# First pair by banks A, B, D, C; short units' operands at the end of their slots; one wait and one turn moved into the first unit's second half

## The reference

```
qn = q / (norm(q, over rows) + 1e-6);  kn = k / (norm(k, over rows) + 1e-6)
a  = softmax(kn^T @ qn / tau)                  # 256 x 256, for each of B = 2 batches
x  = v @ a                                     # 12032 rows of 256
x  = (sigmoid(x @ w_gate) * (x @ w_val)) @ w_out    # d_ff = 1536
h  = x @ w2_in                                 # d_ff = 2048
out = (h - tanh(h)) @ w2_out
```

## Time and profile before

| | before |
|---|---|
| three runs | 2207.38, 2208.68, 2209.26 us, median 2208.68 |
| the profiled execution's own time | 2208.35 us |
| its span, first to last instruction | 2206.4 us |
| granted TensorE clock, mean | 0.999 |
| PE busy | 2189.4 us (99%) |
| VectorE, ScalarE, GpSimd busy | 1549.3, 1276.1, 1153.4 us |
| DMA traffic | 439.46 MB |

### The profile page before, as it was taken

The page is one execution under the profiler, slowest core; times in us unless marked ns, Lnnn a source line. Parts: engine busy times, 40 slices in busy tenths (PEclk is TensorE's granted clock), DMA queues, the critical chain, the costliest instruction groups (busy, mean ns, idle before and its releaser), DMA issues.

```text
span 2206.4 us, 33618 instructions
## 1 busy us (share of the span) xinstructions
PE 2189.4 (99%) x11664; PEld 1908.3 (86%) x11664; DVE 1549.3 (70%) x2933; ACT 1276.1 (58%) x2336; POOL 1153.4 (52%) x970
## 2 busy tenths in 40 slices
PE   8999999999999999999999999999999999999998
PEld 6887988888888898899998898888888889889998
DVE  6879866866775776686586586586586677577566
ACT  5644664665565565565565465465466456556555
POOL 3475653564465464365374365356356446446434
PEclk9999999999999999999999999999999999999999
DMA  9988476476367357457557547546536536635644
GB/s 335 323 284 316 168 218 224 141 237 210 127 211 241 125 182 227 169 178 237 199 187 228 185 168 222 175 140 216 191 134 212 185 134 202 207 124 182 232 143 151
DMA packets 286473, 439.46 MB, mean 199 GB/s; under 512 B 208096, under 2 KB 214496, under 8 KB 286304
## 3 DMA queue, kind: packets, MB, share of 16 engines
q1 hardware_dynamic: 279184, 409.82, 56.5%
q0 software_dynamic: 5264, 27.27, 3.2%
q10 hardware_dynamic: 1856, 0.23, 0.1%
HBM read 386.14 MB, written 51.12 MB: 198 GB/s over the span
## 4 chain that ended last, share of the span: by engine, by line
PE 95%; DMA 2%; POOL 1%; DVE 1%; issue 1%; ACT 0%; SPq 0%; ACTq 0%; DVEq 0%; POOLq 0%
PE up L1610 53%; PE x_acc L1610 21%; PE acc L1610 19%; PE x_acc L1636 3%; DMA qk_in<-in_k 1%; DMA w_sums<-g 0%; POOL g L694 0%; POOL g L689 0%; DVE g_lo L1323 0%; POOL vt_lo L705 0%; POOL vt_hi L705 0%; POOL x_lo L705 0%; POOL g L687 0%; SPq L438 0%; ACT g L877 0%
## 5 line engine op out<-in xcount | busy, mean ns | idle before, releaser
L739 POOL TENSOR_TENSOR g<-t_sums,g 128x512 fp32r<-128x512 f32 (+1 forms) x384 | 502.5, 1325 | 371.1 <-ACT g L1026 371.0
L729 POOL TENSOR_TENSOR g_lo<-func_out,g_hi 128x512 fp32r<-128x512 f32 (+1 forms) x253 | 313.8, 1269 | 570.6 <-ACT g_hi L961 570.4
L1610 PE MATMUL up<-vt_hi,ring 128*128 128x512 f32 (+1 forms) x1848 | 562.6, 386 | 0.0
L1610 PEld LDWEIGHTS up<-vt_hi,ring 128*128 128x128 f32 x1848 | 347.3, 188 | 62.8
L1610 PE MATMUL up<-vt_lo,ring 128*128 128x512 f32 (+1 forms) x924 | 358.5, 388 | 0.3
L1336 DVE TENSOR_TENSOR held<-up,held 128x512 f32<-128x512 f32 (+1 forms) x132 | 89.7, 679 | 366.8 <-PE up L1610 366.8
L1026 ACT ACTIVATE g<-t_sums 128x512 fp32r<-128x512 f32 (+1 forms) x384 | 237.8, 619 | 157.2 <-DVE t_sums L1419 156.9
L1610 PE MATMUL x_acc<-g,ring 128*128 128x256 f32 (+1 forms) x2304 | 304.4, 282 | 0.0
L1610 PE MATMUL up<-x_lo,in_w_hi 128*128 128x512 f32 (+1 forms) x768 | 298.3, 388 | 1.1 <-DVE x_lo L1379 1.1
L1610 PE MATMUL up<-x_hi,in_w_lo 128*128 128x512 f32 (+1 forms) x768 | 297.7, 388 | 0.0
L1610 PE MATMUL up<-x_hi,in_w_hi 128*128 128x512 f32 (+1 forms) x768 | 296.2, 386 | 0.0
(11 more groups left out here) (258 smaller groups left out, 3617.3 us busy)
## 6 DMA issues: line engine op xcount, KB each, us to landing
ring<-w_sums SPq DMA_DIRECT2D x192, 896.0 KB, 4.6
ring<-u_records SPq DMA_DIRECT2D x132, 896.0 KB, 6.1
d_ring<-d_records SPq DMA_DIRECT2D x70, 512.0 KB, 6.3
qk_in<-in_q SPq DMA_DIRECT2D x29, 384.0 KB, 4.5
qk_in<-in_k SPq DMA_DIRECT2D x29, 384.0 KB, 6.0
u_records<-g POOLq DMA_DIRECT2D x12, 896.0 KB, 10.7
v_in<-in_v SPq DMA_DIRECT2D x160, 64.0 KB, 2.4
out_rows<-out_sb SPq DMA_DIRECT2D x160, 64.0 KB, 2.2
```

What stands on the lines that cost most here:

```text
L729: pool.tensor_tensor(g1_lo[:, i, 0:w], func_out[:, i, 0:w], g1_hi[:, i, 0:w].bitcast(F32), ALU.subtract).then_inc(g_lo_made, 2 if last and ...
L739: pool.tensor_tensor(lo[:, cut, 0:half], t_sums[:, first - T1:first - T1 + 2, 0:half], hi[:, cut, 0:half].bitcast(F32), ALU.subtract).then ...
L1610: mm = pe.matmul(psum, a, b, start=start and n == 0, stop=stop and n == 2, skip_group_check=shared_bank)
```

## The change

The banks of the first pair are taken in the order A, B, D, C, on all engines: VectorE's products, ScalarE's high parts, GpSimd's low parts, and the opening of the next pair's gate on TensorE, which becomes M1, M6, M5, M7, M2 in place of M1, M5, M6, M7, M2. In a short unit the operands that TensorE streams (v, x of both blocks, g) lie in the last 448 (or 224) columns of their slots; the columns that the other engines read from and the PSUM columns stay. The turn of the second half of v for unit 1 goes from step j = 10 of unit 0's first half to pair k = 1 of its second half. The wait for `u_s_stored[5]` goes from before the second half to `hi_of_vt_sums(0, 1)`, at k = 13, which is what overwrites the staged parts.

```diff
+    def tail(w):
+        return slice(W - w, W)
+    def half_tail(half):
+        return slice(W // 2 - half, W // 2)
...
-    FIRST_ORDER = [A_, D_, C_, B_]
+    FIRST_ORDER = [A_, B_, D_, C_]
...
+    SEAM_M6, SEAM_M5 = 2, 3
...
-        NEXT_V_TURNS = [3, 10]
+        FIRST_V_TURN, LATE_V_TURN = 3, 1
...
-                sp.dma_start(v_in[g * Q:(g + 1) * Q, h, 0:w // Q, :],
+                sp.dma_start(v_in[g * Q:(g + 1) * Q, h, TB - w // Q:TB, :],
...
-                    pool.tensor_tensor(g1_lo[:, i, 0:w], func_out[:, i, 0:w],
-                                       g1_hi[:, i, 0:w].bitcast(F32), ALU.subtract
+                    pool.tensor_tensor(g1_lo[:, i, tail(w)], func_out[:, i, 0:w],
+                                       g1_hi[:, i, tail(w)].bitcast(F32), ALU.subtract
... (the same for g1_hi, x2_hi, x2_lo with tail(w), and for the parts of g2 with half_tail(half))
             def hi_of_vt_sums(t, n):
                 act.wait_ge(vt_summed, 4 * (t + 1))
+                if t == 0 and n == 1:
+                    act.wait_ge(u_s_stored[FOLDS - 1], 32)
...
                 hi_of(t, 0, A_, w)
+                hi_of(t, 0, B_, w)
                 hold_a(gate_steps, gate_copied, n + 1, w, val_summed, 4 * n)
                 hi_of(t, 0, D_, w)
-                hold_d(gate_steps, gate_copied, n + 1, w, val_summed, 4 * n)
+                hold_d(gate_steps, gate_copied, n + 1, w, val_summed, 4 * n, SEAM_M5)
                 hi_of(t, 0, C_, w)
-                hi_of(t, 0, B_, w)
...
             act.wait_ge(u_a_stored, 16 * 8 * FOLDS)
-            for n in (FOLDS - 2, FOLDS - 1):
-                act.wait_ge(u_s_stored[n], 32)
+            act.wait_ge(u_s_stored[FOLDS - 2], 32)
...
+                    if first and k == LATE_V_TURN:
+                        turn_v(1, 1, first=True)
...
-                add_gate(n + 1, w)
+                add_gate(n + 1, w, m6=SEAM_M6)
...
-                if j in NEXT_V_TURNS:
-                    turn_v(1, NEXT_V_TURNS.index(j), first=True)
+                if j == FIRST_V_TURN:
+                    turn_v(1, 0, first=True)
...
                 u_product(gate_steps, i, "M1", w)
-                pe.wait_ge(prod_made, 4 * (n - 1) + order.index(D_) + 1)
-                u_product(gate_steps, i, "M5", w)
-                pe.wait_ge(prod_made, 4 * (n - 1) + order.index(B_) + 1)
-                u_product(gate_steps, i, "M6", w)
+                if p == 1:
+                    pe.wait_ge(prod_made, 4 * (n - 1) + order.index(B_) + 1)
+                    u_product(gate_steps, i, "M6", w)
+                    pe.wait_ge(prod_made, 4 * (n - 1) + order.index(D_) + 1)
+                    u_product(gate_steps, i, "M5", w)
+                    pe.wait_ge(prod_made, 4 * (n - 1) + order.index(C_) + 1)
+                else:
+                    (M5, then M6, as before)
                 u_product(gate_steps, i, "M7", w)
...
-                product3(up[bank_no][:, 0:w], both(weights, ALL, a), both(VT, ALL, b, slice(0, w)),
+                product3(up[bank_no][:, 0:w], both(weights, ALL, a), both(VT, ALL, b, tail(w)),
... (the same for D and P_ with tail(w), for O with half_tail(half))
```

More of the change, by code:

```diff
@@ L738, in lo_of_t @@
                     pool.wait_ge(t_hi_made, 2 * (BOTH * t + k) + (first - T1) // 2 + 1)
-                    pool.tensor_tensor(lo[:, cut, 0:half], t_sums[:, first - T1:first - T1 + 2, 0:half],
-                                       hi[:, cut, 0:half].bitcast(F32), ALU.subtract
+                    pool.tensor_tensor(lo[:, cut, half_tail(half)],
+                                       t_sums[:, first - T1:first - T1 + 2, 0:half],
+                                       hi[:, cut, half_tail(half)].bitcast(F32), ALU.subtract
                                        ).then_inc(t_lo_made, 1)
@@ L923, in hold_a, with hold_d @@
                 act.activation(held[:, HELD_A, 0:w], up[A_][:, 0:w], ACT.Copy).then_inc(copied, 1)
-            def hold_d(steps, copied, n, w, other_summed, other_done):
-                act.wait_ge(steps, PRODUCTS * n + M5)
+            def hold_d(steps, copied, n, w, other_summed, other_done, m5=M5):
+                act.wait_ge(steps, PRODUCTS * n + m5)
                 if other_done is not None:
@@ L1015, in hi_of_g @@
                 act.wait_ge(g_made, n + 1)
-                act.activation(hi[:, G11, 0:half], even[:, 0:half], ACT.Copy).then_inc(p_hi_made, 1)
+                act.activation(hi[:, G11, half_tail(half)], even[:, 0:half], ACT.Copy).then_inc(p_hi_made, 1)
                 act.wait_ge(g_made, n + 2)
-                act.activation(hi[:, G21:G22 + 1, 0:half],
+                act.activation(hi[:, G21:G22 + 1, half_tail(half)],
                                odd[:, 0:w].rearrange("p (o c) -> p o c", o=2), ACT.Copy
@@ L1025, in hi_of_t @@
                 act.wait_ge(t_sums_made, 4 * (BOTH * t + k) + first - T1 + 2)
-                act.activation(pair_part(k, HI)[:, cut, 0:half],
+                act.activation(pair_part(k, HI)[:, cut, half_tail(half)],
                                t_sums[:, first - T1:first - T1 + 2, 0:half], ACT.Copy
@@ L1350, in add_up, with add_gate @@
                                       ).then_inc(summed, 1)
-            def add_gate(n, w, first=False):
+            def add_gate(n, w, first=False, m6=M6):
                 add_up(gate_steps, gate_copied, gate_summed, n, w, val_summed,
-                       None if first else 4 * n, True)
+                       None if first else 4 * n, True, m6)
             def add_val(n, p, w):
@@ L1414, in sums_and_lo_of_pair @@
                                   ).then_inc(t_sums_made, 1)
-                dve.tensor_tensor(lo[:, G11, 0:half], g11, hi[:, G11, 0:half].bitcast(F32),
+                dve.tensor_tensor(lo[:, G11, half_tail(half)], g11,
+                                  hi[:, G11, half_tail(half)].bitcast(F32),
                                   ALU.subtract).then_inc(p_lo_made, 1)
@@ L1425, in sums_and_lo_of_pair @@
                                   ).then_inc(t_sums_made, 1)
[L1426 removed]
+                dve.tensor_tensor(lo[:, G21:G22 + 1, half_tail(half)],
                                   odd[:, 0:w].rearrange("p (o c) -> p o c", o=2),
[L1428 removed]
+                                  hi[:, G21:G22 + 1, half_tail(half)].bitcast(F32), ALU.subtract
                                   ).then_inc(p_lo_made, 1)
@@ L1711, in down @@
                     mm = product3(x2_banks[s][h][:, 0:w], both(weights, ALL, cols(h)),
-                                  both(G1, ALL, blk, slice(0, w)), first, last)
+                                  both(G1, ALL, blk, tail(w)), first, last)
                     if last and h == 0:
@@ L1824, in P_ @@
                     mm = product3(up[bank_no][:, 0:w], both(WIN, ALL, kc, cols(i)),
-                                  both(X2, ALL, s, kc, slice(0, w)), kc == 0, kc == KC - 1)
+                                  both(X2, ALL, s, kc, tail(w)), kc == 0, kc == KC - 1)
                 mm.then_inc(p_made, 1)
@@ L1844, in o_products @@
                         pe.wait_ge(t_lo_made, 2 * (BOTH * t + k) + 2)
-                    mm = product3(psum, both(weights, ALL, a), both(g, ALL, b, slice(0, half)),
+                    mm = product3(psum, both(weights, ALL, a), both(g, ALL, b, half_tail(half)),
                                   m == 0 and opens, m == PAIRS - 1, shared_bank=True)
```

16 lines of the change are left out of this document (8 added, 8 removed).

## The result

| | before | after |
|---|---|---|
| median of 10 runs, us | 2208.77 (2207.38 to 2210.31) | 2203.81 (2200.77 to 2205.49) |
| after / before, 95% interval | | 0.9977 (0.9969 to 0.9985) |
| the profiled execution's own time, its span | 2208.35, 2206.4 | 2205.16, 2203.2 |

The profiled execution of the new kernel lies 1.35 us above its median, so what the two traces differ by, 3.2 us, is less than what the medians differ by, 5.0.

What follows compares the result with a forecast made beforehand. TensorE, busy 99% of the span, was taken as the bound, so only its waits and matmul distances count. 2208.35 - 3.5 - 1.9 + 0 = 2202.95, stated as 2203.1 us toward the runs' median, range 2197.0 to 2206.0.

Steps and rivals of the forecast that it cites:

- part 3: Short units' operands at the end of their slots: 0 us, the middle of -2.7 to +2.0 around today's mixture.
- Part 1: Order A, B, D, C at the first pair: TensorE's wait for B's product goes, 0.32 us a unit, -3.5 us.
- Part 2: End of unit 0's first half: two waits go with the turn and store wait moved, P starts at 210.41, -1.9 us.
- (a): First pair: ScalarE's copy of D starts later, VectorE's sums still end 0.5 us before the gate's M4; cost 0.
- (b): First pair: `D(t, 0, 1)` wants GpSimd's fourth low part instead of the third, margin 0.5 us; cost 0.
- The rule weighed there: End of unit 0's first half: DMA costs about 2.0 us plus bytes at 436 GB/s; forecast went by the trace's 4.3 us.
- Where the pieces land: Turn behind pair k = 1, where VectorE idles, and wait at k = 13, 70 us behind the store's landing: both cost 0.
- The bounds of -9.0 and +25.5: Short operands' matmuls: best case 200.0 and 106.7 ns, -9.0 us; worst, a short one costs 226.7 ns, +25.5 us.
- A: Rival: the place in the slot helps, 448s run at 200 ns; 2194 to 2200.4 us, say 2197; chance 0.20.
- B: Rival: the place in the slot slows the 448s to 209.6 ns or over, up to 2228.6 us; chance 0.04.
- C: Rival: the wait at the pair's turn only changes its name, TensorE stands one product later; 2206.5 us; chance 0.11.
- D: Rival: something else holds the copy of x at 210.6, only the first 0.5 us goes; 2204.4 us; chance 0.09.

Runs made afterwards that it cites:

- e5: The changed kernel once more, unaltered, on another run; 2203.77 us, ratio 0.9978 to the kernel before.
- e6: The changed kernel with the short units' operands back at the start of their slots; 2203.62 us, ratio 0.9978 to the kernel before.
- e1: The kernel before with only the new order of banks A, B, D, C; 2206.74 us, ratio 0.9987.
- e2: The kernel before with only the turn of v moved from j = 10 to k = 1 of the second half; 2208.51 us, ratio 0.9993.
- e3: The kernel before with only the wait for the last store moved to k = 13; 2207.36 us, ratio 0.9993.
- e4: The kernel before with only the short units' operands moved to the end of their slots; 2208.06 us, ratio 0.9996.
- e10: The kernel before with only the half-width operands of O (parts of g) at the end of their slots; 2208.62 us, one run.
- e11: The kernel before with only the 448-column operands at the end of their slots, those of O at the start; 2208.17 us, one run.
- e9: The changed kernel with operands at the start of their slots and the ring load issued ahead of the loads of v; 2203.35 us, ratio 0.9972 to the kernel before.
- e7: The changed kernel with the ring load of pair 1's value records issued ahead of the eight loads of v; 2203.90 us, ratio 0.9980 to the kernel before.

## Why the prediction was right, and where its account was not

2203.1 us was forecast, with 2197.0 to 2206.0 around it; the medians are 2203.81 for the changed kernel, 2203.77 for the same again (e5) and 2203.62 without part 3 (e6). Parts 1 and 2 were right in mechanism and in size. Part 3 and the closeness of the total owe something to luck, as told below.

- **Part 1, -3.5.** -3.50 by the account, -3.6 in e1. It was right for the reason given: the earlier trace rows showed the jump at M6, the four products in order, and only B's was the last. In detail the full-width units gave 0.32 to 0.36, the short ones (5 and 11) 0.2, unit 6 0.48, of which 0.13 came right behind the pair, where a weight load no longer waits 0.3 us for VectorE's sum. Margins (a) and (b) held with 0.54 and 0.58 us.
- **Part 2, -1.9.** -1.90 with the restart. P starts at 210.76 and not at 210.41, because this execution came out of the first stage 0.37 us later: the difference is to be read, not the time of day. The first low part of x (209.63, about 0.69 us) ends near 210.3, 0.4 us ahead of P, the margin given. e2 and e3 show both halves of the argument, that the store held `x_hi` and that the turn alone gives nothing.
- **The rule weighed there.** The store took 4.3 us in the earlier trace rows and 4.3 to 4.4 in after, e2 and e3. The estimate by the Trainium skill ("DMA: Bandwidth & Descriptors", section "Anatomy of one DMA") was 3.2 us for it, and 0.6 us for all of part 2. The measurement differs from it and decides: e3 alone gave 1.3 us by moving that wait. But the rule was asked for more than it says. That section is headed as the path of DMAs that GpSimd issues, it is about one DMA by itself, and this store, issued by SyncE, stood 0.56 us behind another of the same size. That other one, in the trace of before, landed 3.1 us after its issue, close to the 3.2:

```profile
u_records<-vt_hi SPq DMA_DIRECT2D x1, 512.0 KB, 3.1
```

  After, e2 and e3 have the same pair, 3.1 and then 4.3 or 4.4. So what the estimate most likely left out is the store in front; no run moved the two apart.
- **Where the pieces land.** Both at no cost: no weight load of the kernel after waits at k = 1 to 3 or at k = 13.
- **Part 3, 0.** -0.52 in the second halves by the account, inside the levels given. The reason, "the middle of the two levels", was only a bet. Whether the place also cost something in the first halves (the +0.8 of wider distances) isn't settled: see the last section. In the medians the whole of part 3 doesn't show (e5 against e6, 0.15 us apart, known to about 1.8 us either way). The bounds of -9.0 and +25.5 were far wider than what any place did.
- **Not in the sum.** +0.37 in the first stage, +1.6 ring waits, about +0.8 wider distances. With them and the -0.52 the sum gives the profiled execution: 2202.95 + 0.37 + 1.59 + 0.84 - 0.52 = 2205.23, and it took 2205.16. They are read from this same trace, so that it closes is no test. The median lies 1.35 us below that, so part of them falls on this one execution; how much of them an average one has, the runs don't show. That the forecast, which had none of these terms, came so near the median is partly luck. The 0.7 us between forecast and median is no more than the ratio's interval leaves open (1.8 us to either side).

Of the rivals, **A** (200 ns or less) isn't seen: the least mean over a half is 203.0 ns, and over the 12 matmuls of one P 202.5. **B** fell: no half is near 209.6. **C** fell by the list of waits. **D** fell by ScalarE's row at 209.00. Its price was wrong too: with the copy still held, it counted the first wait as 0.5 us won, where e2 shows 0.16, so it should have stood near 2204.7.

No version beats the kernel after by more than its scatter.

## What to carry to other kernels

When several products in a row leave for an engine that wants them in turn, look which of them depends only on work already done, and send that first; a list of identical short waits, one a unit, is the sign. Where two waits end near one another, the trace of before shows only what each costs in the other's presence: find what each is released by, since taking the earlier one away alone gives nothing. And below some 1.5 us, read the difference of the n-th instructions' starts, not the span: the first stage and the loads moved the span by as much as a part of the change.

## What the runs showed of the hardware

**Two distances in one loop.** In the first halves of units 5 and 11 the 448s follow one another at a mean of either about 202.7 or 206.7 ns, and change from one to the other in the course of a half. The kernel after had 206.7 nearly all through unit 11's, from the chain in order of time:

```profile
2053.30 3.10 PE up L1622 x15
```

In e4, with the same operands and places, it is the other one early in that half:

```profile
2056.85 3.04 PE up L1619 x15
```

The means over the 396 matmuls of these halves, distances over 215 ns (waits) left out, unit 5 / unit 11:

| order of banks | operands at the start | operands at the end |
|---|---|---|
| as before | before 205.7 / 204.4, e2 205.9 / 205.7, e3 203.0 / 203.2, e10 205.9 / 204.5 | e4 203.8 / 203.8, e11 205.7 / 203.8 |
| A, B, D, C | e1 203.0 / 206.3, e6 205.1 / 203.7, e9 205.0 / 203.0 | after 206.3 / 206.3, e5 205.7 / 206.3, e7 205.4 / 206.3 |

The same kernel gives nearly the same picture twice (after and e5), and the new order with the operands at the end has high means in all three traces, where the same order with the operands at the start has a low one in each. With the old order the end is no worse than the start. So the edit may have a part in it, and two to four traces for each case don't decide it. A half is worth up to 1.6 us (396 x 4 ns), so this could have taken back what part 3 won in the second halves.

At the lower level in unit 11 the weight loads stand idle for 49 to 54 ns once every 13.4 us, where 10 to 19 ns between two of them are usual. Eight traces (before, e2, e3, e4, e6, e9, e10, e11) have 29 of these, and the change to 206.7 comes within 0.8 us behind the last one of each trace; behind the other 21 nothing changes, and in e1, after, e5 and e7 the level rises without one. So these holds mark places at which it can change; that they cause it isn't shown, and what the level depends on stays open.

**What goes before sets the next ones' distance.** 205.0, 204.2 and 203.5 ns for P with O's operands at the start, in the middle (where P's own place matters as well) and at the end of their slots; half-width matmuls of 224 columns themselves are 111.2 ns apart in all 13 traces.

**Loads behind other DMAs of the same queue.** At the start of a unit's first half SyncE needed from 7.3 to 13.5 us to issue the eight loads of v, over all traces; the eight of the same unit's later part took 4.0 to 5.2. Ring loads that held TensorE in the chains landed 5.3 to 7.1 us after their own issue. The wait of the matmul at 1021.59, 1.3 us by the account, is well inside that spread.
